# Attention and two mixture layers on one core: the order of loads, stores and GpSimd's work around the attention stage and the first products

## The reference

```python
scores = (1/sqrt(64)) * q @ k.T          # q, k, v: (4, 12, 448, 64)
scores = cap * tanh(scores / cap)        # cap = 30
attn = exp(scores - max) / sum           # the kernel leaves the max out
x = (attn @ v), heads side by side       # 1792 tokens x 768
h = maximum(maximum(x @ w1, x @ w2), x @ w3) @ moe_w_out
g = h @ w_gate; out = (g * sigmoid(g) * (h @ w_val)) @ moe2_w_out   # d_ff 1536
```

## Time and profile before

| | us |
|---|---|
| median of 3 runs | 992.14 |
| the runs | 989.82, 998.17, 992.14 |
| the profiled execution | 990.72 |
| its span, first to last instruction | 988.9 |
| PE busy | 981.1 (99%) |
| DVE busy | 745.9 (75%) |
| POOL busy | 650.3 (66%) |
| ACT busy | 530.8 (54%) |

### The profile page before, as it was taken

One profiled execution on the slowest core, in us unless ns is written; L12 is line 12 of the kernel. 1 busy time (PEld: TensorE's weight loads), 2 busy tenths in 40 slices (PEclk: granted clock), 3 DMA queues, 4 the chain that ended last, 5 costly groups with the idle time before them and its releaser, 6 DMA issues. The chain is left out here.

```text
span 988.9 us, 14171 instructions
## 1 busy us (share of the span) xinstructions
PE 981.1 (99%) x4678; PEld 822.2 (83%) x4678; DVE 745.9 (75%) x938; ACT 530.8 (54%) x950; POOL 650.3 (66%) x592
## 2 busy tenths in 40 slices
PE   9999999999999999999999999999999999999998
PEld 5555555569999999999999999999999999999997
DVE  5999999983867798885378896657589888238884
ACT  7899998853433455544355454334355554335540
POOL 4568889788998567656466486565475765656651
PEclk9999999999999999999999999999999999999999
DMA  7899998998755333335533885333333333643345
GB/s 224 258 294 299 296 292 278 307 310 264 218 173 171 102 112 112 108 109 154 174 112 105 298 279 168 106 112 105 103 116 94 118 107 92 197 142 109 108 146 174
DMA packets 125800, 174.16 MB, mean 176 GB/s; under 512 B 14240, under 2 KB 122656, under 8 KB 125728
## 3 DMA queue, kind: packets, MB, share of 16 engines
q1 hardware_dynamic: 125728, 173.26, 56.5%
HBM read 133.79 MB, written 39.42 MB: 175 GB/s over the span
## 5 line engine op out<-in xcount | busy, mean ns | idle before, releaser
L632 POOL TENSOR_TENSOR w_lo<-whole,w_hi 128x384 fp32r<-128x384 f32 x420 | 473.6, 1152 | 254.7 <-ACT w_hi L800 254.7
L741 PE MATMUL acc<-a_hi,w_hi 128*128 128x448 f32 x882 | 323.2, 366 | 0.3
L741 PE MATMUL acc<-a_hi,w_lo 128*128 128x448 f32 x882 | 322.8, 366 | 0.0
L741 PE MATMUL acc<-a_lo,w_hi 128*128 128x448 f32 x882 | 322.7, 366 | 0.0
L800 ACT ACTIVATE w_hi<-whole 128x384 fp32r<-128x384 f32 x420 | 201.2, 515 | 73.1 <-DMA whole<-w_in 42.8
L741 PEld LDWEIGHTS acc<-a_hi,w_hi 128*128 128x128 f32 x882 | 165.6, 188 | 16.3 <-ACT p L822 0.9
L741 PEld LDWEIGHTS acc<-a_lo,w_hi 128*128 128x128 f32 x882 | 165.6, 188 | 14.1
L741 PEld LDWEIGHTS acc<-a_hi,w_lo 128*128 128x128 f32 x882 | 165.6, 188 | 13.9
L813 ACT ACTIVATE b_hi<-b_whole 128x448 fp32r<-128x448 f32 x126 | 70.5, 575 | 158.8 <-DVE b_whole L1012 65.8
L693 PE MATMUL acc<-prob,v_one 128*128 128x448 f32 (+1 forms) x384 | 141.8, 559 | 0.5 <-ACT prob L795 0.2
L597 POOL TENSOR_TENSOR raw_w<-raw_w 128x384 f32<-128x384 f32 x96 | 102.6, 1069 | 56.9 <-DMA raw_w<-w_in 51.3
(11 more groups left out here) (74 smaller groups left out, 990.7 us busy)
## 6 DMA issues: line engine op xcount, KB each, us to landing
whole<-s_store SPq DMA_DIRECT2D x240, 192.0 KB, 2.4
whole<-w_in SPq DMA_DIRECT2D x180, 192.0 KB, 2.4
raw_w<-w_in SPq DMA_DIRECT2D x24, 768.0 KB, 6.7
s_store<-raw_w SPq DMA_DIRECT2D x24, 768.0 KB, 8.3
qk_raw<-qk_in SPq DMA_DIRECT2D x23, 480.0 KB, 5.7
part_store<-sig SPq DMA_DIRECT2D x24, 224.0 KB, 3.0
sig<-part_store SPq DMA_DIRECT2D x24, 224.0 KB, 3.6
out<-sig SPq DMA_DIRECT2D x24, 224.0 KB, 2.9
```

What stands on the lines that cost most here:

```text
L632: nc.gpsimd.tensor_tensor(w_lo[:, n % RING, :], whole[:, n % RING, :], w_hi[:, n % RING, :].bitcast(F32), ALU.subtract).then_inc(w_lo_done, 1)
L741: last = nc.tensor.matmul(bank(q, BANK_OF[i]), w[:, n % RING, cols], m[:, i, c, :], start=(i < 4 and c == 0 and t == 0), stop=(c == KCH - ...
```

## The change

SP loads queries and keys of pair g+3 in step g (of pair 2 and 3 in step 0), so it waits for the split of pair g+1. It stores the sums of pair g-1 ahead of the x stores of the step; the sums of 22 are stored among the last x stores, those of 23 at product 6. The first late load waits for the stores of 21 and 22 alone. POOL starts the sums of pair g (to 21) only when DVE has split pair g+2; the sums of 22 come after the steps, and those of 23 one at a time after `weights_lo` 10 to 13. Late sums follow `weights_lo` 13 + 11k/5 instead of 13 + 2k; their stores lie at products 12, 21, 30, 39, 47 and 56 instead of 12, 20, 28, 36, 44 and 52. At quad 8, DVE waits for the third late buffer two results later. ACT takes p1 ahead of the operand that waits for a stage's last difference, and ahead of the first casts of the x loaded back. On DVE, at a stage's start one operand low moves behind u4, and in quads 27 and 28 the lows of x loaded back move behind the additions.

```diff
 LATE_SUMS = QUADS - EARLY_SUMS
 LATE_RAWS = 3
 LATE_FROM = AHEAD + 3
-LATE_STEP = 2
 LATE_LOAD = 2
-LATE_STORE = 12
+LAST_STORE = 6
+def late_after(k):
+    return LATE_FROM + 11 * k // 5
+LATE_STORE = [late_after(4 * i + 3) - (AHEAD - 3) for i in range(LATE_SUMS)]
 X_SPLIT_FROM = 3
...
             for g in range(ALL_PAIRS):
                 if g + 2 < ALL_PAIRS:
                     load_v(g + 2)
-                    load_qk(g + 2)
+                if g == 0:
+                    load_qk(2)
+                if g + 3 < ALL_PAIRS:
+                    load_qk(g + 3)
                 if RING_FROM <= g < RING_FROM + RING:
                     load_weights(g - RING_FROM)
                 if g + 1 < EARLY_SUMS:
                     load_raw(g + 1)
+                if 1 <= g < ALL_PAIRS - 1:
+                    store_sum(g - 1)
                 for c, j in later_stores(g):
                     store_x(c, j)
-                if g >= 1:
-                    store_sum(g - 1)
             assert sorted(later_stores(ALL_PAIRS)) == sorted((KCH - 1, j) for j in LAST_STORES)
-            for j in LAST_STORES[:2]:
-                store_x(KCH - 1, j)
-            store_sum(ALL_PAIRS - 1)
-            for j in LAST_STORES[2:-LAST_MADE]:
+            store_x(KCH - 1, LAST_STORES[0])
+            store_sum(ALL_PAIRS - 2)
+            for j in LAST_STORES[1:-LAST_MADE]:
                 store_x(KCH - 1, j)
             for q in range(ALL_QUADS):
                 kind, g, f = kind_of(q)
...
                     if m == LATE_LOAD:
                         sp.wait_ge(value_done, STEPS)
                         sp.wait_ge(norm_done, ALL_PAIRS)
-                        for n in range(RAWS):
-                            sp.wait_ge(sum_stored[n], 16 * EARLY_SUMS // RAWS)
+                        for i in (ALL_PAIRS - 3, ALL_PAIRS - 2):
+                            sp.wait_ge(sum_stored[i % RAWS], 16 * (i // RAWS + 1))
                     if 0 <= m - LATE_LOAD < LATE_RAWS:
                         load_late(m - LATE_LOAD)
-                    late, moment = divmod(m - LATE_STORE, 4 * LATE_STEP)
-                    if 0 <= late < LATE_SUMS and moment == 0:
-                        store_late(late)
-                    if 0 <= late < LATE_SUMS - LATE_RAWS and moment == 3:
-                        load_late(late + LATE_RAWS)
+                    if m == LAST_STORE:
+                        store_sum(ALL_PAIRS - 1)
+                    if m in LATE_STORE:
+                        store_late(LATE_STORE.index(m))
+                    if m - 3 in LATE_STORE[:LATE_SUMS - LATE_RAWS]:
+                        load_late(LATE_STORE.index(m - 3) + LATE_RAWS)
                     if kind == "out" and g > 0 and i == 0:
                         load_part(q, 3)
                         load_part(q, 0)
...
                                 (a11, a22, a11, ALU.subtract), (a12, a12, a11, ALU.subtract))[n]
                 nc.gpsimd.tensor_tensor(to, x, y, op).then_inc(done, 1)
+            def early_sum(i, n):
+                if n == 0:
+                    pool.wait_ge(raw_loaded[i % RAWS], 16 * (i // RAWS + 1))
+                sum_of_weights([raw_w[:, i % RAWS, b, :] for b in range(4)], n, 4 * i, sum_done)
             def early_sums(i):
-                pool.wait_ge(raw_loaded[i % RAWS], 16 * (i // RAWS + 1))
                 for n in range(4):
-                    sum_of_weights([raw_w[:, i % RAWS, b, :] for b in range(4)], n, 4 * i, sum_done)
+                    early_sum(i, n)
             def late_sum(k):
                 i, n = divmod(k, 4)
...
                 for cols in ones_cols:
                     nc.gpsimd.memset(v_one[:, b, cols], 1.0).then_inc(ones_done, 1)
             for g in range(ALL_PAIRS):
-                if g < ALL_PAIRS - 1:
+                if g + 2 < ALL_PAIRS:
+                    pool.wait_ge(qk_split, g + 4)
                     early_sums(g)
                 if 0 <= g - LO_FROM < FIRST_HI:
                     weights_lo(g - LO_FROM)
+                if g == ALL_PAIRS - 1:
+                    later_difference(KCH - 1, 0)
                 if x_split(g - 1) is not None:
                     x_lo(*x_split(g - 1))
-                if g >= LATER + 3:
+                if LATER + 3 <= g < ALL_PAIRS - 1:
                     c, i = divmod(g - LATER - 3, 4)
                     for which in ((0,), (1, 2), (3,), ())[i]:
                         later_difference(c, which)
-            early_sums(ALL_PAIRS - 1)
+            early_sums(ALL_PAIRS - 2)
             later_difference(KCH - 1, 1)
             later_difference(KCH - 1, 2)
             x_lo(*x_split(ALL_PAIRS - 1))
             later_difference(KCH - 1, 3)
             for n in range(FIRST_HI, PROD * ALL_QUADS):
                 weights_lo(n)
-                k, moment = divmod(n - LATE_FROM, LATE_STEP)
-                if 0 <= k < 4 * LATE_SUMS and moment == 0:
-                    late_sum(k)
+                if n < FIRST_HI + 4:
+                    early_sum(ALL_PAIRS - 1, n - FIRST_HI)
+                for k in range(4 * LATE_SUMS):
+                    if n == late_after(k):
+                        late_sum(k)
         @block.tensor
         def _(pe):
...
                         operand_hi(made, 2)
                     if i == 0 and urgent:
                         operand_hi(made, 5)
+                    if i == 0:
+                        take_p1(q)
+                    if i == 0 and urgent:
                         operand_hi(made, 6)
                     if q == K_OUT21 and i == 0:
                         for _ in range(X_CASTS[q, i]):
                             operand_hi(*loaded.pop(0))
-                    if i == 0:
-                        take_p1(q)
                     if made is not None and i == 1 and not urgent:
                         operand_hi(made, 3)
                         operand_hi(made, 4)
...
                 if n == 0 and event_of(q) == KCH * ST_H:
                     for i in range(RAWS):
                         dve.wait_ge(sum_stored[i], 16 * EARLY_SUMS // RAWS)
-                elif n == 0 and event_of(q) == KCH * (ST_H + 1) - 1:
-                    for i in range(LATE_RAWS):
+                elif n in (0, 2) and event_of(q) == KCH * (ST_H + 1) - 1:
+                    for i in (range(LATE_RAWS - 1) if n == 0 else range(LATE_RAWS - 1, LATE_RAWS)):
                         dve.wait_ge(late_stored[i], 64 * LATE_SUMS // LATE_RAWS)
             def tmp_free(q, n):
...
                 last = e is not None and e % KCH == KCH - 1
                 if q == QUADS:
                     some_of_left(X_LEFT - 3)
-                else:
-                    some_of_left(len(left) if q % QUADS in STARTS else 1)
-                if q == K_OUT21:
-                    left += [(KCH * STAGES + c, n, j) for n, (c, j) in enumerate(X_AGAIN)]
-                    some_of_left(X_CASTS[q, 0])
+                elif q % QUADS in STARTS:
+                    some_of_left(len(left) - 1)
+                elif q != K_OUT21 + 1:
+                    some_of_left(1)
                 add_u2(q)
-                if q not in (K_OUT21, QUADS):
+                if q % QUADS not in STARTS and q != K_OUT21 + 1:
                     some_of_left(1)
                 add_u4(q)
-                if q not in (K_OUT21, QUADS):
-                    some_of_left(1)
+                if q != QUADS:
+                    some_of_left(2 if q == K_OUT21 + 1 else 1)
                 add_c22(q)
                 if q == QUADS:
                     some_of_left(len(left))
                 elif not K_OUT21 <= q < QUADS:
                     some_of_left(2)
                 add_c11(q)
+                if q == K_OUT21:
+                    left += [(KCH * STAGES + c, n, j) for n, (c, j) in enumerate(X_AGAIN)]
+                    some_of_left(X_CASTS[q, 0])
+                elif q == K_OUT21 + 1:
+                    some_of_left(1)
                 if kind == "gate":
                     gate_of(q, 0)
                     gate_of(q, 1)
...
                     gate_of(q, 2)
                     gate_of(q, 3)
                 if K_OUT21 <= q < QUADS:
-                    some_of_left((1, 1, len(left) - X_LEFT)[q - K_OUT21])
+                    some_of_left((0, 1, len(left) - X_LEFT)[q - K_OUT21])
                 elif e is None:
                     some_of_left(len(left))
     return nc
```

## The result

The changed kernel takes 1003.66 us in the median (990.52 to 1006.12, 22 executions), the kernel before 992.18 on the same chip (983.86 to 1007.81, 22): 11.5 us slower. The ratio, 1.0078 [1.0046, 1.0111], leaves out executions more than 1.5% above the fastest of their kernel (four after, one before); the medians alone give 1.0116. Forecast were 988.0 and a range from 984 to 994. The profiled execution after took 991.17 us, close to the fastest, span 989.4.

What follows compares the result with a forecast made beforehand. PE, busy 99%, bounds the kernel, so only holes in its stream can be won: 2.98 + 0.73 + 0.44 = 4.15 us, taking the profiled 990.72 to 986.6; median forecast 988.0 us, range 984 to 994.

Steps and rivals of the forecast that it cites:

- The cost of pushing GpSimd back: Later sums, stores and loads; last sums between w_lo 10 to 13 leave about 9 of 12.6 us spare: nothing.
- The rule: Shared DVE and GpSimd port is taken for a whole instruction; each split instruction could wait out one of 1.14 us.
- Attention, 2.98 us: Holes in PE's stream between late pairs, from late loads and port sharing together; counted as won in full.
- Splits of 0.65 and 1.16 us: Sign of being right: DVE's cast and subtract of queries and keys take their times beside an idle GpSimd.
- the first rival: Tails of GpSimd's steps block DVE's splits in steps 15 to 21: 4.3 us of holes, 992.3 us; chance 0.12.
- the three I counted: GpSimd tails, in steps 15, 16 and 20, long enough to reach into a split; 2.0 us for the three, DVE's lead 4.0.
- the two parts I had credited together: Queries loaded a pair further ahead and GpSimd behind DVE's split, together credited with the 2.98 us.
- ScalarE and DVE order, 0.73 + 0.44: Product stages: bank 0 copied earlier saves 0.37 + 0.36; DVE's two lows no longer before its additions save 0.44.
- the hole near 299: Hole in the products not touched by the change: 0, or 0.39 us if GpSimd is less in the way.
- the five that I counted: Holes said to be left in the 3780 matmuls of the product stages.
- the raw ring: Three raw blocks must close in 25.5 us and need 23: nothing on PE; rival that it fails, 996, chance 0.07.
- It matters for the runs and not for the change: Wider matmul spacing from about 763 us, 0.004 us each, 4.3 us in the profile, 15 over all 3780 matmuls.

Runs made afterwards that it cites:

- pacing: Changed kernel with GpSimd making w_lo 14 to 61 only when product n-5 is done: 989.79 us, ratio 0.9966 [0.9926, 1.0007], span 980.8.
- breaking once: Changed kernel with one wait more, w_lo 14 only when product 9 is done: 989.98 us, one execution.
- The kernel with the sums alone: Kernel before with only pair 23's sums one at a time after w_lo 10 to 13, store at product 6: 1004.28 us, ratio 1.0081.
- the one with the hole and DVE's other order: Changed kernel, GpSimd not paced, DVE's order mended with only the last low of quads 12 and 42 behind the third addition: 992.16 us, ratio 1.0032.
- a third with a hole at 1872 and an edge at 813: Paced kernel, DVE's order mended but only the last low of quads 12 and 42 behind the third addition: 991.79 us, ratio 0.9976.
- the five kernels made to try this: DVE's order mended, paced: 984.33 us; plus two reciprocals: 988.25; quad 10 put back: 984.11; only the last low moved: 991.79; that without pacing: 992.16.
- putting the edge at 675 back: Paced kernel with DVE's mended order, quad 10 alone put back as in the changed kernel: 984.11 us, ratio 0.9885 [0.9850, 0.9920].
- Paced GpSimd with the cleared order: Changed kernel, GpSimd paced, DVE's differences or lows moved in quads 10, 12, 28, 40, 42: 984.33 us, ratio 0.9895; quad 10 put back: 0.9885.
- filler kernels: Not the kernel: trains of GpSimd subtracts without a gap, with DVE instructions asking at chosen points; output is filler, no kernel time.

## Why the prediction was wrong, point by point

**The failed step is "The cost of pushing GpSimd back".** It put the last sums between `weights_lo` 10 to 13 and priced them at "Nothing, hidden by this lead", looking only at whether weights would be late. They were not. What the step did not ask is what a GpSimd without rest does to DVE. The wait of 2.69 us for the late load in the kernel before looked like idle time of an engine off the path; it ended the train in which DVE would else have been shut out. Price: 0 in the prediction, 8.6 us measured, shown by adding the part alone and by removing it, pacing, or breaking once.

**The rule was weighed with the wrong range.** The Trainium skill, "SBUF — State Buffer", section "Who interferes with whom", says that a DVE instruction with two SBUF inputs contends with GpSimd and that the second to issue blocks fully. I took this as one GpSimd instruction of 1.14 us at most, and weighed it for the splits alone, not for the products. Up to some 14 GpSimd instructions in a row the runs agree with that (0.62 to 1.47 us for an instruction of 0.62); beyond, DVE waited out 16 of them. The page also has copies contend, and not an instruction with one SBUF input that is outside the two-port modes; the copy (7.82) and the reciprocal (2.95, as in the attention stage) agree. The section speaks of no wait longer than one instruction.

**Attention, 2.98 us: right in size, half right in its reason.** "Splits of 0.65 and 1.16 us" did not come: the last ten subtracts of the kernel after still stand beside GpSimd, as here.

```profile
193.12 0.64 DVE L941 CAST qk_hi<-qk_raw 128x960 fp32r<-128x960 f32 x1
193.80 1.98 DVE L943 TENSOR_TENSOR qk_lo<-qk_raw,qk_hi 128x960 fp32r<-128x960 f32 x1
```

The tails of the first rival reach into most late splits, more than the three I counted. But casts are back at 0.64 in all but two of them, no split waits for its load, and 2.62 us instead of 3.55 leave DVE its lead. The first rival's price (4.3 us of holes) did not come. Of the two parts I had credited together, the wait for the split does it alone (every pair 8.49 apart with the old load, 1.1 us lost without the wait).

**ScalarE and DVE order, 0.73 + 0.44: right**, and the hole near 299 closed too (0.39, in my bound). The trace of before has four holes in the products, those at 299.58, 377.16, 581.30 and 761.02, not the five that I counted. The loads, stores and the raw ring cost nothing, as forecast.

**"It matters for the runs and not for the change" was wrong.** I took the wider spacing as a lottery outside the kernel. The change came with other odds. Why is argued only: it took away the visible late holes, at which a wide stretch can become narrow again, and put a hole at matmul 171. Neither is the whole of it. The kernel with the sums alone kept the holes at 804 and 2694 and is as slow (1004.28), and the one with the hole and DVE's other order stayed narrow in seven of twelve (992.16). Thirteen of 22 executions after lie 11.7 us or more above the narrow time. Groups at +8, +12.5 and +14.5 are what turns at matmuls 1818, 675 and 171 would give (7.9, 12.4, 14.4), and the profile after has these three released 0.17, 0.17 and 0.06 us before their start. It has three more late ones: 822, 2565 and 2712 (0.28, 0.18, 0.28 us). A turn at 2712 gives +4.3, where the one at 994.8 stands; 2565 would give +4.9.

**What is shown and what is open.** Shown: the shut-out, its counting and its cause in the moved sums; that turns of the spacing lie at late releases or holes, in the ten profiles that have one. The traces say it more exactly. The narrow spacing is a sequence of five distances repeated, 0.207, 0.202, 0.203, 0.202 and 0.199 us, the wide one 0.206 to 0.207 throughout. Every turn to the wide one begins exactly at such a matmul: 675 in three profiles, 2703 in two (the turns at "about 2709"), 171, 810, 1818, 1872, 2565 and 2712 in one each. Argued only: that late releases cause the turns. Moving edges did move the groups (two versions 1% faster on six executions each, a third with a hole at 1872 and an edge at 813 not), but the text's exact groups came in none of the five kernels made to try this, and putting the edge at 675 back brought no group of its own. A direct trial with a matmul that has nothing else near it was not made, and which executions turn can't be told beforehand. Nor is shown why the count is near 14, or what differs between a 32-column and a 448-column admission.

**Beating both.** Paced GpSimd with the cleared order is 1.1% faster than the kernel before (0.9885 and 0.9895), at six executions each and on a chip where the kernel before had a median of 996.77, against 992.18 on the chip of the result. Of the gain, 4 us are the forecast parts; the rest is spacing, by the profiles because it falls back to narrow at a small hole.

## What to carry to other kernels

When a change lets one engine run without rest, ask what the rests were for: look on DVE for two-operand SBUF instructions beside the longest gapless run of GpSimd, and break that run before the fourteenth instruction. A wait of GpSimd for its own last result was enough (0.08 us). An instruction that takes 16 us instead of 0.6 is found by its length, not by sums of busy time, where it is 1.6% of the span. Where executions of one kernel stand in groups, divide the distances by the per-instruction difference that two profiles show; the quotient tells where in the program the kinds of execution part.

## What the runs showed of the hardware

- A DVE instruction with two SBUF operands, or a copy from SBUF, that asks after 15 or more GpSimd instructions without a gap waits until GpSimd rests (after 14, two of five did): 16.30, 15.86, 16.58, 16.28 us in four kernels, up to 15.50 in the filler kernels. The count is of instructions (shut out 9.9 us into a train of short ones, let in at 12.5 us of long ones). A rest of 0.08 us, that of a wait for its own result, resets it, so does a full-length DVE admission on the way; a satisfied wait and a 32-column admission do not.
- PE spaced the same 448-column matmuls 0.2027 or 0.2067 us apart on average at a granted clock of 1.00, for a thousand of them and more, and turned from one to the other only at late releases and holes in these fifteen profiles.
- Behind a rest of 1.85 us, as behind rests of 6.8 to 7.8, seven to fourteen matmuls came 0.37 us apart, at the 1.2 GHz level (granted clock 0.50); behind the holes of 1.07 us and less none did.
